# Windowed attention ahead of two feed-forward layers: q and k transposed on the host, two key tiles' scores merged into one

## The reference

```
scores = scale * q @ k.T                     # scale = 1/8
is_sink = pos[None, :] < 4
rel = pos[:, None] - pos[None, :]
in_window = (rel >= 0) & (rel < 128)
scores = where(is_sink | in_window, scores, -1e9)
a = exp(scores - max(scores)); a = a / (sum(a) + 1e-9)
out = a @ v
```

## Time and profile before

| | us |
|---|---|
| median of 3 runs | 873.63 (871.59 to 873.88) |
| the profiled execution | 872.11 |
| its span | 870.4 |
| TensorE busy in the span | 819.3 (94%) |
| first scores | at 11.39 |
| last row of x written by the attention | at 156.6 |
| slots of the experts and dense layer | from 200 to the end |

### The profile page before, as it was taken

How to read it: one execution, slowest core, us unless ns; L and a number is a source line. 1 busy time by engine, 2 the same in 40 slices (tenths; PEclk the granted TensorE clock), 3 DMA queues, 4 the chain that set the end, 5 groups by cost and what they waited for, 6 DMA issues and landing times.

```text
span 870.4 us, 13607 instructions
## 1 busy us (share of the span) xinstructions
PE 819.3 (94%) x4264; PEld 669.7 (77%) x4265; DVE 558.9 (64%) x1182; ACT 281.2 (32%) x496; POOL 271.8 (31%) x250
## 2 busy tenths in 40 slices
PE   5998899937999999999999999997999999999998
PEld 4877788425888888888888888876788888888886
DVE  3888888263544554455444554445998888888876
ACT  3544454213031203030301230014555455544443
POOL 5053300008373818255270846463111001000000
PEclk9999999957999999999999999998999999999999
DMA  6547446205443625325171636302000020001001
GB/s 113 128 117 188 103 97 244 73 0 169 135 160 119 217 60 170 120 101 176 53 225 36 208 104 195 109 25 61 25 25 24 25 73 25 1 0 49 1 1 48
DMA packets 77611, 82.71 MB, mean 95 GB/s; under 512 B 43456, under 2 KB 53184, under 8 KB 77568
## 3 DMA queue, kind: packets, MB, share of 16 engines
q1 hardware_dynamic: 58288, 33.79, 13.7%
q10 hardware_dynamic: 14880, 33.95, 12.1%
q0 software_dynamic: 4400, 14.42, 6.0%
HBM read 65.90 MB, written 16.25 MB: 94 GB/s over the span
## 4 chain that ended last, share of the span: by engine, by line
PE 85%; DVE 8%; issue 2%; ACT 2%; DMA 1%; another core or an unknown queue 1%; SPq 0%; DVEq 0%; POOL 0%; ACTq 0%; POOLq 0%
PE bank L1174 19%; PE bank L1185 19%; PE bank L1246 14%; PE bank L1227 13%; PE bank L1062 4%; PE bank L1163 3%; PE bank L1035 2%; PE bank L1048 2%; PE bank L1064 2%; PE bank L1156 2%; PE bank L1020 2%; PE bank L1111 1%; DVE probs L751 1%; DMA q_in<-in_q 1%; PE bank L1102 1%
## 5 line engine op out<-in xcount | busy, mean ns | idle before, releaser
L1174 PE MATMUL bank<-wgt,xT 128*128 x744 | 185.1, 398 | 1.8 <-DVE xT L914 1.8
L1185 PE MATMUL bank<-wgt,hT 128*128 x744 | 186.0, 399 | 0.0
L504 POOL TENSOR_TENSOR wgt<-stage,wgt 128x1024 f32 (+1 forms) x64 | 151.2, 2398 | 109.0 <-ACT wgt L648 109.0
L1174 PEld LDWEIGHTS bank<-wgt,xT 128*128 128x128 f32 x744 | 139.3, 191 | 30.1 <-issue 2.2
L1185 PEld LDWEIGHTS bank<-wgt,hT 128*128 128x128 f32 x744 | 135.1, 188 | 25.9
L648 ACT ACTIVATE wgt<-stage 128x1024 f32 (+1 forms) x64 | 61.6, 1046 | 278.5 <-PE bank L1185 264.5
L1246 PE MATMUL bank<-wgt,gT 128*128 128x512 f32 x576 | 141.7, 396 | 6.6 <-DVE gT L970 6.6
L1227 PE MATMUL bank<-x2T,wgt 128*128 128x512 f32 (+1 forms) x612 | 138.5, 377 | 0.9 <-DVE x2T L952 0.9
L1246 PEld LDWEIGHTS bank<-wgt,gT 128*128 128x128 f32 x576 | 108.8, 190 | 30.5 <-issue 6.1
L1227 PEld LDWEIGHTS bank<-x2T,wgt 128*128 128x128 f32 x612 | 109.9, 188 | 22.1 <-POOL wgt L571 1.1
L920 DVE TENSOR_SCALAR h<-bank 128x512 f32<-128x512 f32 x62 | 42.9, 691 | 65.8 <-PE bank L1174 61.6
(11 more groups left out here) (163 smaller groups left out, 989.0 us busy)
## 6 DMA issues: line engine op xcount, KB each, us to landing
stage<-in_moe_w ACTq DMA_DIRECT2D x48, 512.0 KB, 3.5
stage<-in_moe_w SPq DMA_DIRECT2D x16, 512.0 KB, 6.0
y_dram<-y_sb SPq DMA_DIRECT2D x31, 256.0 KB, 2.2
stage<-in_moe_w_in ACTq DMA_DIRECT2D x8, 512.0 KB, 4.4
stage<-in_moe_w_out ACTq DMA_DIRECT2D x8, 512.0 KB, 3.6
q_in<-in_q SPq DMA_DIRECT2D x16, 192.0 KB, 4.3
v_in<-in_v SPq DMA_DIRECT2D x16, 192.0 KB
x_dram<-x_sb SPq DMA_DIRECT2D x8, 384.0 KB, 5.8
```

What stands on the lines that cost most here:

```text
L504: nc.gpsimd.tensor_tensor(cols(parity, 1, u * UNIT, UNIT), stage[:, u, :], cols(parity, 0, u * UNIT, UNIT).bitcast(fp32), ALU.subtract).th ...
L1174: ins = T.matmul(HA[half][:], xT[:, a, c, :], cols(par, b, c * F + half * 512, 512), start=c == 0 and n == 0, stop=c == NC - 1 and n == 2)
L1185: ins = T.matmul(YB[kk % 2][:], hT[:, a, c, :], cols(par, b, NC * UNIT + c * DM, DM), start=c == 0 and n == 0, stop=c == F // P - 1 and n ...
```

## The change

The host lays q and k out transposed, 128 rows of two heads' 64 dimensions, with the four sink keys beside each key tile, and v with its column of ones; a small array `v_sinks` holds the sinks' values and a row with 1e-9. The transposes of q and k on TensorE go. ScalarE now rounds q and k from SBUF in four pieces a pair (384 columns of q, 396 of k), and VectorE makes their remainders, also from SBUF.

Since every window key of the own tile with a later position than the query is masked and the same column of the tile before is not, the two tiles fill one triangle each. `merge_step` copies the earlier tile's scores over the own tile's where the key is later than the query (`copy_predicated` in PSUM), so a row has 132 columns. The scores carry a negative sign, so that a minimum gives the bias. ScalarE does the exponentials from PSUM on 132 columns, TensorE transposes two blocks and the sinks' block, and ScalarE copies both out (`pT_step`). GpSimd cuts the copied block into the two triangles (`cut_probs`, two selections of 128x256 a unit), and `values` makes one matmul with the sinks and four of 65 columns. Scores now run two units ahead. GpSimd's split of the first expert's weights is woven between the cuts, from unit 14 on.

The pieces of the diff below are, in this order, TensorE's call that goes, GpSimd's cut, ScalarE's loop, VectorE's merge and its loop, and TensorE's value matmuls.

```diff
-                if t <= 2 and not (last and par == 1):
-                    qk_group(i + 1, 1 - par, t)
...
+            def cut_probs(u):
+                b = u % 3
+                pool.wait_ge(pT_ready, u + 1)
+                wait(pool, pv_ready, u - 2)
+                ins = nc.gpsimd.affine_select(out=pT_own[b][:], in_=pT[u % 2][:], compare_op=ALU.is_ge, fill=0.0, base=0,
+                                              pattern=[[0, 2], [1, P]], channel_multiplier=-1)
+                if u % QT > 0:
+                    ins = nc.gpsimd.affine_select(out=pT_prev[b][:], in_=pT[u % 2][:], compare_op=ALU.is_ge, fill=0.0, base=-1,
+                                                  pattern=[[0, 2], [-1, P]], channel_multiplier=1)
+                ins.then_inc(pT_cut, 1)
...
+                    hp, par, t = at_unit(it, n)
+                    if not (last and n + 1 >= 2 * QT):
+                        pT_step(*at_unit(it, n + 1))
+                    if not (last and n + 2 >= 2 * QT):
+                        exp_step(*at_unit(it, n + 2))
+                    if t < 4 and not (last and par == 1):
...
+                        round_qk(par1, t)
...
+                own, prev = OWN[b], PREV[b]
...
+                    V.copy_predicated(own, heads(later[:].bitcast(u32)), prev).then_inc(merged, 1)
+                dve.wait_ge(merged, MERGES[t] + PER_PAIR * (2 * hp + par) + 1)
...
+                V.tensor_reduce(rt["nb"][:, 2 * b:2 * b + 2], SC[b][:, :, SEC:2 * SEC], AX.X, ALU.min).then_inc(bias_ready, 1)
+
+            def qk_remainder(hp, par, piece):
+                dve.wait_ge(qk_rounded, 4 * (2 * hp + par) + piece + 1)
...
+                    hp, par, t = at_unit(it, n)
+                    if not (first and n < 2):
+                        norm_step(*at_unit(it, n - 2))
+                    if not (last and n + 2 >= 2 * QT):
+                        merge_step(*at_unit(it, n + 2))
+                    if t < 4 and not (last and par == 1):
+                        hp1, par1, _ = at_unit(it, n + QT)
+                        qk_remainder(hp1, par1, t)
...
+                T.matmul(OB[b][:, 0:2 * VW], pT_sink[t % 3][:], v_sink[par][:].rearrange("p h d -> p (h d)"), start=True, stop=False)
+                pe.wait_ge(pT_cut, u + 1)
+                for back in ((0,) if t == 0 else (0, 1)):
                     for hd in range(2):
...
+                        ins = T.matmul(OB[b][:, hd * VW:(hd + 1) * VW], (pT_prev if back else pT_own)[t % 3][:, hd, :],
+                                       v_in[par][:, t - back, hd, :], start=False, stop=hd == 1 and (t == 0 or back == 1))
```

More of the change, by code:

```diff
@@ L348, in attention_moe_mish, with qk_split, at_unit @@
+        def qk_split(par, piece, part):
+            if piece % 2 == 0:
+                return qT[par][:, part, piece // 2 * HALF:(piece // 2 + 1) * HALF]
+            return kT[par][:, part, piece // 2 * KHALF:(piece // 2 + 1) * KHALF]
+        def at_unit(it, n):
+            return it + n // QT // 2, n // QT % 2, n % QT
+        MERGES = [0]
+        for t in range(QT):
+            MERGES.append(MERGES[t] + 1 + (t == 1) + (t > 0 and window < P))
+        PER_PAIR = MERGES[QT]
         FIRST = 3
@@ L610, in body @@
+            for piece in range(4):
+                act.wait_ge(qk_first[piece], 16)
+                round_qk(0, piece)
+            exp_step(0, 0, 0)
+            exp_step(0, 0, 1)
+            act.wait_ge(masks_ready, 1)
+            pT_step(0, 0, 0)
             def body(it):
@@ L791, in body @@
+            V = nc.vector
+            for piece in range(4):
+                qk_remainder(0, 0, piece)
+                if piece == 1:
+                    dve.wait_ge(masks_ready, 1)
+                    merge_step(0, 0, 0)
+            merge_step(0, 0, 1)
             def body(it):
                 last = isinstance(it, int) and it == NP // 2 - 1
+                first = isinstance(it, int) and it == 0
                 for n in range(2 * QT):
-                    i, t = 2 * it + n // QT, n % QT
@@ L1069, in _ @@
             scores(0, 0, 0)
+            scores(0, 0, 1)
+            turn_probs(0, 0, 0)
             def body(it):
                 last = isinstance(it, int) and it == NP // 2 - 1
+                first = isinstance(it, int) and it == 0
                 for n in range(2 * QT):
[L1074 to L1078 removed]
@@ L1079, in body @@
-                    turn_probs(i, par, t)
-                    if n >= 1:
-                        values(2 * it + (n - 1) // QT, (n - 1) // QT, (n - 1) % QT)
-                    elif not (isinstance(it, int) and it == 0):
-                        values(2 * it - 1, 1, QT - 1)
+                    if not (last and n + 2 >= 2 * QT):
+                        scores(*at_unit(it, n + 2))
+                    if not (last and n + 1 >= 2 * QT):
+                        turn_probs(*at_unit(it, n + 1))
@@ L1085, in _ @@
+                    if not (first and n == 0):
+                        values(*at_unit(it, n - 1))
             stream_loop(pe, NP // 2, body)
-            values(NP - 1, 1, QT - 1)
+            values(NP // 2 - 1, 1, QT - 1)
             pe.wait_ge(route_consts, 1)
```

435 lines of the change are left out of this document (192 added, 243 removed).

## The result

The changed kernel takes 927.2 us (median of 4 runs, 926.54 to 927.4) against 873.75 us of the kernel before (4 runs, 871.59 to 876.92): 1.061 times as long, 95% interval 1.057 to 1.064. The forecast was 860. The profiled execution has a span of 925.5 us, 55.1 more than before.

The account below looks back on a forecast made before the run. TensorE bounds the kernel now; after the change a VectorE-ScalarE circle of 3.17 us would set the pace. Gains of 7.6 us at the start and 5.4 after it, 13 in all, gave 860 us, range 843 to 876.

Parts of the forecast that it names:

- eight times 0.108 = 0.87 for the 65-column ones: TensorE's value matmuls in the attention: weight load sets each record's time, so eight take 0.87 us despite half the columns.
- 2.49 us a unit: TensorE's own work in a full attention unit: 0.44 transposes, 0.42 sinks, 1.06 values, 0.57 scores.
- 134.3 us to the end: Attention from the third unit's scores: 117 for seven pairs, 14.8 remaining TensorE work, 0.6 last division, 2 collisions.
- the clock: Rival 4, TensorE in the attention: gaps and less occupying records lower its clock; a quarter of units costs 24 us, 884; 12 in 100.
- the circle: Attention units t = 0 to 3: merge, minimum, exponentials, rounding, remainder, division wait on each other, 3.17 us; 52 in 100.
- 65 columns save nothing: Value matmuls in the attention: a 65-column record costs 0.108 us, as one of 130 does, because of its weight load.
- the cuts: GpSimd's 256-column selections in the attention: 0.4 us each, two a unit, hidden behind other TensorE work.
- The collisions: VectorE's two-input SBUF remainders slowed while GpSimd works in the attention: 2 us in all, bounds 0 to 8.
- The start: Start of the attention: larger q rows and no transposes bring the third unit's scores to 9.3 us, 7.6 earlier.
- the records' spacing: Sign in TensorE's trace: 65-column records at 0.108 us from start to start.
- PEclk is below 0.95: Sign of being wrong: the clock column in the attention reads below 0.95.
- The last x near 143: Sign at the attention's end in the changed trace: the last x comes near 143 us.

Follow-up runs that it names:

- the late remainders: Changed kernel with VectorE's q/k remainders one unit later, so they no longer wait for their own unit's rounding: 928.18 us, ratio 1.061.
- the fall at 62 us: Clock drop in the changed kernel with remainders one unit later and 24 transposes added once inside the loop: 910.99 us, one run.
- the added matmul: Changed kernel plus one 260-column fp32 matmul a unit, identity times v into unused columns, output unused: 923.15 us, one run.

## Why the prediction was wrong

**The failed step** is the one that took all of TensorE's durations at full level: "eight times 0.108 = 0.87 for the 65-column ones" and with it 2.49 us a unit. The records took 0.22 to 0.23 and the unit 4.42. The sum itself holds at full level, where the same unit took 2.49; what failed is that TensorE would be at that level. From the third unit's scores on, the prediction had 134.3 us to the end; the trace has 9.28 to 210.94, 201.7. The difference, 67.4, is that between forecast and measurement (927.2 less 860). The rival was named: the clock, priced at 4.8 us a unit (measured 4.42, since at half rate nobody waits). What failed in it is its extent and its chance. It assumed that the waits lose the clock, for "a quarter" of the units, 884 us, 12 in 100. Here all 48 units were at half rate, with 0.4 us of waits, and the four executions lie within 0.9 us of each other. The kernel before has the wide records and came back within some 3 us of its one long wait; I took that recovery for granted in a kernel whose records are different.

**That this is the cause** is shown for the width: the two pairs of kernels that differ only in it, both with the sinks last, lie 52.6 and 73.4 us apart, and in the narrow ones the level is low throughout the attention. That the circle's waits are not the cause is shown by the late remainders (928.18, nothing gained), and by the fall at 62 us without a wait. Not shown: what share the removed transposes have, and which property of a record it is that keeps the level. The Trainium skill, "TensorE: Matmul & The Clock Gate", section "Part 4: PE-mode transpose", which the prediction weighed, says that full clock doesn't engage for transposes, which don't count as busy in the same way. The runs disagree in one respect: 14 transposes and nothing else brought the full level within 3.2 us. That two added transposes a unit kept it for 25 us only, and the added matmul for 65, would fit the Trainium skill, but these are single runs. The prediction drew from the same section of the Trainium skill that the share of work that counts would fall; but four transposes a unit were removed, which by that rule raises the share unless waits come in, and there were 0.4 us of waits.

**65 columns save nothing:** right at full level (0.93 to 1.01 against 0.98 for eight). The prediction ended the thought there, and named a narrow record only as one that might keep TensorE less occupied. The pairs above show that the loss hangs on this width; by what property is not shown.

**The circle:** right, and hidden by the slower clock. With the clock up its steps measured: merge 0.43 (forecast 0.43, its bounds were 0.29 and 0.69), minimum 0.43 (0.43), the two exponentials 0.35 each (0.45 for both, measured 0.60 to 0.63: too low), rounding 0.52 alone (0.56, of which 0.50 shows), remainder 0.56 (0.55), sum 3.0 to 3.1 (3.17). The kernel that has it with the clock up takes 859.66 us and begins routing at 145.5, where the prediction had 860 and the last x near 143. That the totals agree is in part luck: a half-rate stretch of about 7 us, which the prediction's sum doesn't have, is partly offset by a circle some 3 us cheaper over its 28 units, and the kernel compared is not the changed one but its wide form with the sinks last and added transposes at the start. The circle's 3.0 and TensorE's 2.49 and 2.47 are the firm parts.

**GpSimd:** the cuts take 0.41 (forecast 0.4) and are hidden. The collisions are real: a remainder takes 0.55 to 0.57 alone and up to 1.39 while GpSimd works (VectorE, then GpSimd, changed kernel):

```profile
124.99 1.39 DVE L783 TENSOR_TENSOR kT<-k_in,kT 128x396 fp32r<-128x396 f32 x1 [1.31 <-ACT kT L590]
```

```profile
124.69 1.27 POOL L484 TENSOR_TENSOR wgt<-stage,wgt 128x512 fp32r<-128x512 f32 x1
```

In all the 28 remainders lost 11 us (means of 846 and 1065 ns instead of 560), 3.5 in the kernel with the clock up and the circle in it (698 and 669); forecast 2, bounds 0 to 8. At half rate none of it reaches TensorE. The slower remainders beside GpSimd agree with the Trainium skill, "GPSIMD Engine Reference", section "Specifications", which the prediction cited with no row to show it. That a remainder lasts over 1 us there was one of the signs of being wrong, and it came true without mattering.

**The start:** right. The third unit's scores begin at 9.28 (forecast 9.3), 7.6 us earlier than before.

**Behind the attention** nothing moved, as forecast: the shift of 55.1 us at routing's start is the shift of the end.

**The signs named in advance:** the records' spacing was the sign that worked. "PEclk is below 0.95" did not: the column read 1.00 throughout, and the runs suggest that it starts from full and shows only changes that the trace recorded. "The last x near 143" failed too (it came at 211.4).

## What to carry to other kernels

Where the weight load sets a matmul's duration, halving its streamed columns saves little or no time and can cost TensorE its clock: here 52.6 and 73.4 us in two pairs of kernels. Before pricing such an edit, price each record at both levels, and read the level from the spacing of equal records, not from the clock column alone. A measured recovery after a wait belongs to the work that recovered; with other records it has to be measured again.

## What the runs showed that I had not expected

- A TensorE that is busy 100% of 196 us can stay at the lower level for all of it (88 records in 20 us), and fall to it from the full level with no wait at all (at 62 us).
- Doing more work is faster: the 130-column form computes twice the needed output in its value matmuls and is 52.6 and 73.4 us faster than the 65-column form; 23 added transposes take another 6 us off (840.95 to 834.71).
- 14 to 24 transposes in a row bring the full level; they do not make the narrow form keep it.
- How fast the full level comes back after a wait depends on the work: about 3 us in the kernel before, 14 to 17 with its value matmuls at 65 columns, 17 and 20 with wide ones but without the q/k transposes.
- The clock column showed 1.00 where the records ran at half rate, until the first recorded change.
- A two-input VectorE instruction on SBUF went from 0.56 to 1.39 us beside GpSimd; the 128x256 predicated copy in PSUM took 0.43 us.
